# Attention units as two halves of 64 tokens in a fused attention and two-layer MLP kernel

## The reference

```python
B, H, S, D = q.shape
f = 1.0 / (1.0 + np.exp(-f_logit))
state = np.zeros((B, H, D, D), dtype=np.float32)
for t in range(S):
    state = f[:, :, t, :, None] * state + np.einsum('bhd,bhe->bhde', k[:, :, t], v[:, :, t])
    y[:, :, t] = np.einsum('bhd,bhde->bhe', q[:, :, t], state)
x = y.transpose(0, 2, 1, 3).reshape(B * S, H * D)
x = softplus(x @ w_in) @ w_out        # max(h, 0) + log1p(exp(-|h|))
h = x @ w2_in                         # second layer
out = np.where(h >= 1, h, np.where(h <= -1, 0.0, (h + 1) ** 2 / 4)) @ w2_out
```

## Time and profile before

| | |
|---|---|
| median of 3 runs | 919.57 us (918.11 to 922.22) |
| profiled execution | 920.22 us, span 918.3 us |
| TensorE busy | 898.0 us (98%) |
| VectorE, ScalarE, GpSimd busy | 512.9, 446.4, 67.3 us |
| chain that ended last | 92% TensorE |

### The profile page before, as it was taken

How to read it: one execution, slowest core, us unless ns; L and a number is a source line. 1 busy time by engine, 2 the same in 40 slices (tenths; PEclk the granted TensorE clock), 3 DMA queues, 4 the chain that set the end, 5 groups by cost and what they waited for, 6 DMA issues and landing times.

```text
span 918.3 us, 14986 instructions
## 1 busy us (share of the span) xinstructions
PE 898.0 (98%) x5810; PEld 742.0 (81%) x5810; DVE 512.9 (56%) x875; ACT 446.4 (49%) x839; POOL 67.3 (7%) x59
## 2 busy tenths in 40 slices
PE   7889999999999999999999999999999999999996
PEld 4789988888888888888888888888888888888884
DVE  5976765566555555654355655555555555555453
ACT  5876665565565555665577533232332332333222
POOL 2112211111111111110000100000000000000000
PEclk9999999999999999999999999999999999999999
DMA  8622222112111311400033200200200200200001
GB/s 276 208 80 65 84 70 74 43 42 77 43 42 54 96 55 42 149 33 1 23 116 98 75 1 1 69 1 1 70 1 0 69 1 1 70 1 10 25 1 37
DMA packets 22300, 50.57 MB, mean 55 GB/s; under 512 B 2384, under 2 KB 3152, under 8 KB 22224
## 3 DMA queue, kind: packets, MB, share of 16 engines
q1 hardware_dynamic: 22224, 49.55, 17.2%
HBM read 40.11 MB, written 9.44 MB: 54 GB/s over the span
## 4 chain that ended last, share of the span: by engine, by line
PE 92%; DVE 2%; ACT 2%; issue 1%; DMA 1%; POOL 1%; SPq 0%; DVEq 0%
PE h_ps L458 15%; PE h_ps L460 14%; PE h_ps L459 14%; PE y_ps L458 14%; PE y_ps L460 14%; PE y_ps L459 14%; PE a_ps L514 2%; PE c_ps L528 1%; PE a_ps L557 1%; PE c_ps L540 1%; PE c_ps L547 1%; PE c_ps L532 1%; PE c_ps L502 1%; DMA qkf_sb<-qkf 1%; POOL qkf_sb L433 1%
## 5 line engine op out<-in xcount | busy, mean ns | idle before, releaser
L818 DVE TENSOR_TENSOR g_lo<-gate,g_hi 128x512 fp32r<-128x512 f32 (+1 forms) x208 | 135.2, 650 | 355.3 <-ACT g_hi L664 354.4
L458 PE MATMUL h_ps<-x_hi,w_hi 128*128 128x512 f32 (+1 forms) x624 | 237.9, 381 | 4.4 <-issue 2.1
L458 PE MATMUL y_ps<-g_hi,w_hi 128*128 128x512 f32 (+1 forms) x624 | 233.4, 374 | 3.5 <-DVE g_lo L818 3.5
L459 PE MATMUL h_ps<-x_lo,w_hi 128*128 128x512 f32 (+1 forms) x624 | 232.8, 373 | 0.0
L460 PE MATMUL h_ps<-x_hi,w_lo 128*128 128x512 f32 (+1 forms) x624 | 232.7, 373 | 0.0
L460 PE MATMUL y_ps<-g_hi,w_lo 128*128 128x512 f32 (+1 forms) x624 | 232.6, 373 | 0.0
L459 PE MATMUL y_ps<-g_lo,w_hi 128*128 128x512 f32 (+1 forms) x624 | 232.5, 373 | 0.0
L652 ACT ACTIVATE soft<-h_ps 128x512 f32<-128x512 f32 x96 | 57.4, 598 | 266.1 <-PE h_ps L460 265.0
L648 ACT ACTIVATE soft<-h_ps 128x512 f32<-128x512 f32 (+1 forms) x112 | 60.0, 536 | 169.7 <-PE h_ps L460 169.7
L458 PEld LDWEIGHTS h_ps<-x_hi,w_hi 128*128 128x128 f32 x624 | 117.3, 188 | 29.4 <-issue 4.7
L458 PEld LDWEIGHTS y_ps<-g_hi,w_hi 128*128 128x128 f32 x624 | 117.4, 188 | 25.9 <-DVE g_lo L818 5.3
(11 more groups left out here) (76 smaller groups left out, 619.1 us busy)
## 6 DMA issues: line engine op xcount, KB each, us to landing
w_raw<-w SPq DMA_DIRECT2D x32, 384.0 KB, 6.0
qkf_sb<-qkf SPq DMA_DIRECT2D x24, 448.0 KB, 4.5
v_sb<-v SPq DMA_DIRECT2D x24, 256.0 KB, 4.5
qkf_sb<-qkf SPq DMA_DIRECT2D x24, 224.0 KB, 3.0
qkf_sb<-x_mid SPq DMA_DIRECT2D x6, 768.0 KB, 5.5
out<-y_sb SPq DMA_DIRECT2D x18, 256.0 KB, 2.2
x_mid<-y_sb SPq DMA_DIRECT2D x15, 256.0 KB, 2.3
x_mid<-y_sb SPq DMA_DIRECT2D x6, 128.0 KB, 1.9
```

Source lines behind the costliest of these rows:

```text
L458: nc.tensor.matmul(out_ap, hi1, hi2, start=start, stop=False, skip_group_check=True)
L459: nc.tensor.matmul(out_ap, hi1, lo2, start=False, stop=False, skip_group_check=True)
L818: nc.vector.tensor_tensor(g_lo[:, t % 2, 0:g.n], gate[:, t % 2, 0:g.n], g_hi[:, t % 2, 0:g.n].bitcast(F32), ALU.subtract).then_inc(glo_don ...
```

## The change

Units 4 to 23 are taken as two halves of 64 tokens. Scores are computed within each half only; what crosses from the first half to the second goes through `mid`, a second state: the state plus the first half's increment. `total` is mid plus the second half's increment, and the next unit's state is total times the decay. Scores use 64x64 tiles of the array (two row halves by two column halves), results 64x32 tiles, eight of them; each row half of the array writes a bank of its own, so the two parts of a result end in two banks (c_ps and b_ps), which ScalarE and VectorE add up (`copy_rows`, `add_x`). The increment of unit u - 1 moves from block 2 to block 1 of unit u, and its results to the slot behind that, so that block 1 is transposes(u), increment(u - 1), scores(u) and block 2 is results(u - 1). `STEP` gives each unit's slot: 17, 20, 23, 26 and 28 for units 4 to 8 (counted over all groups, 16 a group), and then every fourth from 32. In the rows below att_ps is the three banks under one name.

```diff
-MAIN = {2: (7, 12), 3: (3, 7, 11), 4: (0, 4, 8, 12)}
 PREP = (-5, -4, -3, -1)
-STAGES = (0, 1, 2, 3)
-EARLY_STAGES = (0, 1, 3, 4)
-EARLY_STAGES_PE = (0, 2, 3, 4)
+WHOLE = (0, 1, 3, 4)
+WHOLE_PE = (0, 2, 3, 4)
+HALVES = (0, 1, 1, 2, 3)
+HALVES_FAST = (0, 1, 1, 2, 3)
+FAST_STEPS = (1, 4, 7, 10, 12)
 HALF = 32
+REST = D - HALF
 HEAD = 2 * HALF
+T2 = P // 2
...
-def make_slots():
-    out = {}
-    for g in LAYER0[1:]:
-        for j in range(g.count):
-            out[g.unit + j] = FT * (g.index - 1) + MAIN[g.count][j]
+def make_steps():
+
+    out = {2: 7, 3: 12}
+    for u in range(B, UNITS + 1):
+        out[u] = FT + FAST_STEPS[u - B] if u <= 2 * B else 2 * FT + 4 * (u - 2 * B - 1)
     return out
 
 
-MAIN_SLOT = make_slots()
-
-
-def main_at(g, slot, first=EARLY_STAGES):
-    at = FT * g.index + slot
+STEP = make_steps()
+
+
+def main_at(g, slot, whole=WHOLE):
+
     if g.layer:
         return []
-    stages = {u: first if u < 2 * FIRST else STAGES for u in MAIN_SLOT}
-    return [(u, stages[u].index(at - m)) for u, m in MAIN_SLOT.items() if at - m in stages[u]]
+    at, out = FT * g.index + slot, []
+    for u, m in STEP.items():
+        stages = whole if u < B else HALVES_FAST if u <= 2 * B else HALVES
+        out += [(u, s) for s, d in enumerate(stages) if at == m + d]
+    return out
...
-        a_ps = ps("a_ps", [P, 512])
-        b_ps = ps("b_ps", [P, 512])
-        c_ps = ps("c_ps", [P, 512])
+        att_ps = ps("att_ps", [P, 3 * 512])
+        c_ps, a_ps, b_ps = (att_ps[:, 512 * i:512 * (i + 1)] for i in range(3))
...
+        def increment_ps(bank, first=5 * T2):
+            return bank[0:ROWS, first:first + PAIRS * D].rearrange("p (q e) -> p q e", q=PAIRS)
+
+        def result_ps(row_tile, half, k):
+
+            first = (2 * T2, 0)[row_tile] + (KT * half + k) * T2
+            return (c_ps, b_ps)[row_tile][:, first:first + T2]
+
+        def both_halves(row_tile):
+            first = (2 * T2, 0)[row_tile]
+            return (c_ps, b_ps)[row_tile][:, first:first + DM].rearrange("p (n k t) -> p n k t", n=2, k=KT)
...
+                            sp.wait_ge(e_done, u - RING + 1)
+                            load_f(u)
                             unit_left(u - RING)
-                            load_unit(u)
+                            load_qk(u)
+                            load_v(u)
...
+            pool.memset(state[:], 0.0).then_inc(consts, 1)
+            pool.memset(mid[:], 0.0).then_inc(consts, 1)
+            pool.wait_ge(consts, 6)
 
             pool.affine_select(out=causal[:], in_=causal[:], compare_op=ALU.is_ge, fill=0.0, base=0,
                                pattern=[[1, P]], channel_multiplier=-1).then_inc(consts, 1)
             pool.affine_select(out=ident[:], in_=ident[:], compare_op=ALU.not_equal, fill=1.0, base=0,
                                pattern=[[1, P]], channel_multiplier=-1).then_inc(consts, 1)
+            pool.wait_ge(consts, 8)
+            for half in (slice(0, T2), slice(T2, P)):
+                pool.tensor_copy(causal2[half, :], causal[half, half]).then_inc(consts, 1)
+            pool.wait_ge(consts, 10)
...
             def increment(u):
-                a_ps, kt = banks(u)[0], k_tok_of(u)
+                vu = v_sb[:, u % RING].rearrange("p (h e) -> p h e", h=H)
+                pe.wait_ge(k_tok_done, u + 1)
+                pe.wait_ge(v_in[u % RING], 16 * (u // RING + 1))
+                pe.wait_ge(masked, masks_until(u))
                 for p in range(PAIRS):
-                    for a, cols in ((0, slice(0, 64)), (1, slice(64, ROWS))):
-                        h = 2 * p + a
-                        mm = nc.tensor.matmul(a_ps[cols, p * HEAD:(p + 1) * HEAD], kt[:, p, cols],
-                                              v_sb[:, u % RING, h * HEAD:(h + 1) * HEAD],
-                                              start=True, stop=True, skip_group_check=True)
+                    for a in range(2):
+                        for half, bank in ((0, a_ps), (1, b_ps)) if has_future(u) else ((0, a_ps),):
+                            t = slice(half * T2, (half + 1) * T2)
+                            mm = nc.tensor.matmul(bank[64 * a:64 * a + D, 5 * T2 + p * D:5 * T2 + (p + 1) * D],
+                                                  k_tok[t, p, 64 * a:64 * a + D], vu[t, 2 * p + a, data_columns(a)],
+                                                  start=True, stop=True, skip_group_check=True)
                 mm.then_inc(kv_done, 1)
 
+            def score(u):
+                q, k = qkf_sb[:, u % RING, 0], qkf_sb[:, u % RING, 1]
+                pe.wait_ge(q_done, u + 1)
+                pe.wait_ge(masked, masks_until(u - 1))
+                if whole(u - 1):
+                    pe.wait_ge(state_done, u)
+                for p in range(PAIRS):
+                    for half in range(2):
+                        t = slice(half * T2, (half + 1) * T2)
+                        for a, bank in ((0, a_ps), (64, b_ps)):
+                            mm = nc.tensor.matmul(bank[t, (p + 1) * T2:(p + 2) * T2], k[a:a + D, p, t], q[a:a + D, p, t],
+                                                  start=True, stop=True, skip_group_check=True)
+                mm.then_inc(sc_done, 1)
+
+            def result(u):
+                q, sc, vu = qkf_sb[:, u % RING, 0], half_scores(u), v_sb[:, u % RING].rearrange("p (h e) -> p h e", h=H)
+                tokens = (slice(0, T2), slice(T2, P))
+                pe.wait_ge(v_in[u % RING], 16 * (u // RING + 1))
+                pe.wait_ge(masked, masks_until(min(u + 1, UNITS - 1)))
+                pe.wait_ge(k_tok_done, min(u + 2, UNITS))
+                pe.wait_ge(total_done, states_until(u) - B)
+                for a in range(2):
+                    for k, columns in ((2 * a, main_columns(a)), (1, rest_columns(a))):
+                        for j in range(PAIRS):
+                            for half, t in enumerate(tokens):
+                                nc.tensor.matmul(result_ps(half, half, k)[HALF * j:HALF * (j + 1), :], vu[t, 2 * j + a, columns],
+                                                 sc[t, a, j, :], start=(a == 0 and k == 0), stop=False, skip_group_check=True)
+                pe.wait_ge(state_done, u - B + 1)
+                pe.wait_ge(mid_done, u - B + 1)
+                for half, t in enumerate(tokens):
+                    st = state[:, batch(u)] if half == 0 else mid
+                    for main in (True, False):
+                        for j in range(PAIRS):
+                            for a in range(2):
+                                rows = slice(64 * a, 64 * a + D)
+                                first = HEAD * j + (REST + REST * a if main else HEAD - REST if a == 0 else 0)
+                                mm = nc.tensor.matmul(result_ps(a, half, 2 * a if main else 1)[HALF * j:HALF * (j + 1), :],
+                                                      st[rows, first:first + HALF], q[rows, j, t],
+                                                      start=False, stop=True, skip_group_check=True)
+                mm.then_inc(ya_done, 1)
+
             def main(u, s):
-                if s == 0:
-                    turn_keys(u)
-                    score(u)
-                if s == 1:
-                    result(u)
-                    if has_future(u):
-                        increment(u)
+                if whole(u):
+                    if s == 0:
+                        main_whole(u)
+                    if s == 1:
+                        result_whole(u)
+                        increment_whole(u)
+                else:
+                    if s == 0:
+                        pe.wait_ge(xs_done, max(u - B - 1, 0))
+                        if u < UNITS:
+                            if whole(u - 1):
+                                pe.wait_ge(zeroed, 2)
+                            turn_keys(u)
+                        if not whole(u - 1):
+                            increment(u - 1)
+                        if u < UNITS:
+                            score(u)
+                    if s == 2 and not whole(u - 1):
+                        result(u - 1)
...
+                if s == 3 and u > B:
+                    copy_rows(u - 1)
+                if s == 4 and u > B:
+                    act.wait_ge(xs_done, u - B)
+                    split_x(u - 1, sum_of(u - 1))
+
+            def copy_rows(u):
+                g, c = place(u)
+                act.wait_ge(ya_done, u + 1)
+                act.wait_ge(zeroed, 2)
+                if g.G >= 2:
+                    act.wait_ge(h_done, FT * (g.G - 1))
+                nc.scalar.activation(by_half(sum_of(u)), both_halves(1), ACT.Copy).then_inc(one_row, 1)
...
+                if s == 1:
+                    if u < UNITS:
+                        mask(u)
+                    if u > B:
+                        middle(u - 1)
+                if s == 3 and u > B:
+                    add_x(u - 1)
+                if s == 4 and u > B:
```

(28 more changed lines are left out.)

## The result

The changed kernel takes 905.15 us (median of 4 runs, 904.41 to 906.85), the kernel before on the same chip 918.84: a ratio of 0.984, 95% interval 0.9817 to 0.9864. I had said 899.5, with 894 to 918 for eight in ten and 896 to 903 for the forecast's own case: it is faster, but by 5.6 us less than forecast. The profiled execution took 905.68, with a span of 903.7 us: 14.6 less than before, where the sum had 20.9.

What follows compares the result with a forecast made beforehand. TensorE, busy 98% of the span, was taken as the bound. From 920.2 us, shorter attention blocks take 24.3; 0.1 for block corrections, 1.0 VectorE, 2.0 load stall and 0.3 start add back: 899.3, stated 899.5, eight in ten 894 to 918.

Steps and rivals of the forecast that it cites:

- the forecast's own case: Whole kernel: the forecast without its rivals holds, 899.5 us with range 896 to 903; chance 0.52.
- the sum: Whole kernel: profiled 920.2 us, less 24.3 for blocks, plus 0.1, 1.0, 2.0 and 0.3, gives 899.3.
- TensorE bounds, and its stream is what counts: Whole kernel: TensorE is busy 98% of the span, so a change helps by what it shortens there, barring new waits.
- Waits: Group 1: new TensorE waits, 1.0 us for VectorE's late work and 2.0 for a late load.
- Block 1: Transposes, increment and scores on four 64x64 tiles in turn: cost 1.64 us a unit, against 1.68 before.
- 16 rounds of eight at 0.056: Block 2: 128 result records on eight tiles in turn, 0.056 us a round, cost 1.32 against 2.62.
- rival 2: Block 2: at most four tiles work together, 16 rounds more, 18 us or half of it, 917; chance 0.17.
- rival 1: Both blocks: instruction issue sets the pace at 0.0275 us a record, 70 us more, 969; chance 0.12.
- The load of unit 8 and the order on GpSimd: Group 1: unit 8's late-loaded keys run before unit 7's queries on GpSimd, stalling TensorE once by 2.0 us.
- VectorE was to cost 1.0: Group 1: VectorE's chain behind the scores and g_lo held back there, put at 1.0 us (0 to 6).
- rival 3: Group 1: VectorE's chain and the load chain cost 6 us more than taken, 906; chance 0.15.
- Start: Start of the run: memsets ahead of ident take 1.4 us, of which 0.3 is left as cost.

Runs made afterwards that it cites:

- e3: Changed kernel with the same result matmuls reordered so that four tiles follow each other in turn instead of eight: 911.62 us, ratio 0.9911 to the kernel before.
- e2: Changed kernel with each of a unit's 64 result matmuls moving only 32 of its 64 tokens: 903.24 us, ratio 0.9812 to the kernel before.
- e5: Changed kernel with units 4 to 8 stepping at slots 0, 3, 6, 9, 12 of group 1, not 1, 4, 7, 10, 12: 908.96 us, ratio 0.9881.
- e7: Changed kernel with units 4 to 8 stepping at slots 1, 3, 6, 9, 12 of group 1, not 1, 4, 7, 10, 12: 905.94 us, ratio 0.9825.
- e4: Changed kernel with GpSimd multiplying only 8 of 128 columns of each unit's keys and queries: 900.43 us, ratio 0.9765 to the kernel before.
- e12: The changed kernel run once more, without edits: 906.62 us, ratio 0.9858 to the kernel before.

## Why the prediction was right, and where it was wrong

1. **TensorE bounds, and its stream is what counts: right.** The blocks give 20 x 0.105 + 16 x 0.975 + 4 x 0.365 (the last four: 2.455 to 2.09) = 19.2, and all of them read from start to start give 19.2 as well, where the sum had 24.2. Waits and late slots take back 7.0: 6.0 in group 1, 0.5 ahead of it, 0.4 behind. What is left has nothing to do with the change's argument: the first dense matmul starts 0.2 us earlier, and the span ends 6.1 us behind the last dense matmul instead of 8.2 (6.0 to 6.7 in the twelve traces of the experiments; the kernel before has one trace). No run says why. Together 14.6.
2. **Block 1: right,** 1.58 for 1.64. Four tiles of 64 columns a round keep the columns' pace.
3. **"16 rounds of eight at 0.056": mechanism right, size wrong, and this is the step that failed.** Cost 1.64 for 1.32, 0.32 x 20 = 6.4 us, the largest term of the miss. Eight tiles do work together at 7 ns a record (first 32 records; e3 shows that four in turn cost 0.23 a block more), so rival 2 is refuted. But behind them there is a gap of some 0.1 us and then a pace that hardly depends on the columns (e2), 8.35 ns a record at best and 10.8 on average. That is rival 1 in a mild form, with the head start of the queue that it named: its price was reckoned for 27.5 ns and it was to decide from 14.5; at the measured pace it takes a quarter of block 2's gain. I had put it in as all or nothing. The range for this term should have had a case between.
4. **Waits: 7.0 from start to start for 3.0, in part by another cause.** This is the second term that failed. The load of unit 8 and the order on GpSimd: right, 1.3 for 2.0 here, 2.4 in three other runs (e5 and e7 take it away). VectorE was to cost 1.0 and cost most of the rest. I had looked for what is queued behind a waiting instruction and had priced VectorE's instructions as if alone; beside GpSimd they take up to four times as long (e4). This is rival 3's place, at half of its price (6.0 in group 1 for the 3.0 taken; it had 6 more). Of the g_lo waits 1.2 stood ahead of group 1 and came in no other trace; its cause is open.
5. **Start:** 0.3 was taken for the memsets. The first dense matmul comes 0.2 us earlier than before, but at 20.5 us in e12, which is the same kernel, for 19.7: what the memsets cost is smaller than what can be told.

Miss by terms: 6.4 (block 2) - 1.2 (block 1) - 0.2 (other blocks) + 4.0 (waits) - 0.5 (start) - 2.1 (end) = 6.4 of 6.3. That block 2 alone seems to account for the whole is luck, since the other terms cancel. So is a part of the total's closeness: the end's 2.1 us stood in no term.

## What to carry to other kernels

Small tiled matmuls have a second limit beside the columns: count the records between two stretches of long matmuls, give the first 32 or so the array's pace, then a gap of 0.1 us, and the rest the pace measured here (8.35 ns a record at best, 10.8 on average). Before VectorE's work is put into other slots, or one of its operands is moved from PSUM to SBUF, look at what GpSimd does at that moment. Where an engine is behind as a whole, putting one of its results earlier only chooses who waits, and near 2 us a wait on TensorE may be paid twice, by the clock.

## What the runs showed of the hardware

- TensorE's starts: 7 ns a record for 32 records with eight 64x32 tiles in turn, 5 with 32 columns for 64 (28 records in 0.14 us). From the 33rd to the 128th record the mean is 10.8 ns, and 9.7 with 32 columns; the steady stretches run at 8.35 in either. The 25 ns of the Trainium skill, "TensorE: Matmul & The Clock Gate", "Wait — 56ns, not 53.3ns?", cited in the prediction, does not hold between different tiles.
- VectorE's instructions beside a GpSimd multiplication of 1.3 us: with two SBUF inputs, scan 1.53 for 0.40, x_lo 1.61 for 0.55, the state's product 1.42 for 0.35; with one, inv<-inv up to 1.41 for 0.41.
- The granted clock halved for 3 us or more behind ten waits of 1.7 to 3.7 us, and not behind others of 1.7 to 2.4.
